# Two mixtures of experts after a short convolution: the first expert run in two parts, and the first layer of each mixture's first slot written ahead of the tables on TensorE

## The reference

```python
# convolution: x (4, 3584, 192), weight (8, 7), out reshaped to x (14336, 192)
out = np.einsum('hk,bskhg->bshg', w, x_unf)
# first mixture: w1 (8, 192, 1024), w2 (8, 1024, 192)
expert_idx = np.argmax(x @ w_gate, axis=1)
for e in range(E):
    mask = expert_idx == e
    out[mask] = gate_w[mask, None] * (np.maximum(x[mask] @ w1[e], 0.0) @ w2[e])
# second mixture, on the first one's output
noisy_logits = x @ w_gate + np.log1p(np.exp(x @ w_noise)) * noise
top2 = np.argpartition(-noisy_logits, 2, axis=1)[:, :2]
for e in range(E):
    for k in range(2):
        mask = top2[:, k] == e
        out[mask] += top2_w[mask, k, None] * (np.maximum(x[mask] @ w1[e], 0.0) @ w2[e])
```

## Time and profile before

| | |
|---|---|
| median of 3 runs | 1960.8 us (1959.62 to 1962.15) |
| the profiled execution | 1964.21 us, its span 1962.2 us |
| stage 1 | 0 to about 144 us |
| first mixture, second mixture | about 144 to 810 us, about 810 to 1962 us |
| PE busy over the span | 1876.2 us (96%) |
| DVE, POOL, ACT busy over the span | 65%, 49%, 47% |
| granted TensorE clock, mean | 0.982 of 2.4 GHz |

### The profile page before, as it was taken

How to read it: one execution, slowest core, us unless ns; L and a number is a source line. 1 busy time by engine, 2 the same in 40 slices (tenths; PEclk the granted TensorE clock), 3 DMA queues, 4 the chain that set the end, 5 groups by cost and what they waited for, 6 DMA issues and landing times.

```text
span 1962.2 us, 51451 instructions
## 1 busy us (share of the span) xinstructions
PE 1876.2 (96%) x14089; PEld 1821.5 (93%) x14090; DVE 1269.1 (65%) x4251; ACT 914.0 (47%) x2420; POOL 967.7 (49%) x1471
## 2 busy tenths in 40 slices
PE   8977599999999999799999999999999999999998
PEld 6657599999999999799999999999999999999998
DVE  5775488788887887655655655655655655655555
ACT  5543345555555455434444444444444444444444
POOL 4888554444444444444444444444444444444444
PEclk9979799999999999899999999999999999999999
DMA  7634243232332332322222222322322322322221
GB/s 274 230 113 128 74 127 120 89 115 79 117 118 84 116 100 92 103 74 62 81 78 62 85 74 62 104 63 63 102 62 64 96 64 66 97 62 86 78 63 48
DMA packets 113487, 185.23 MB, mean 94 GB/s; under 512 B 21675, under 2 KB 87971, under 8 KB 111287
## 3 DMA queue, kind: packets, MB, share of 16 engines
q1 hardware_dynamic: 73383, 104.53, 17.9%
q0 software_dynamic: 39936, 79.95, 12.6%
q10 hardware_dynamic: 144, 0.49, 0.1%
HBM read 111.34 MB, written 77.66 MB: 96 GB/s over the span
## 4 chain that ended last, share of the span: by engine, by line
PE 81%; issue 5%; DVE 5%; POOL 5%; ACT 1%; DMA 1%; DVEq 1%; ACTq 0%; POOLq 0%; SPq 0%
PE bank L1168 26%; PE bank L1169 12%; PE bank L1151 7%; PE bank L1153 7%; PE bank L1149 7%; PE bank L1152 7%; PE bank L1150 7%; POOL rows_of_mixture L1253 4%; PE bank L1138 2%; PE bank L1012 1%; DVE h_l L857 1%; PE bank L1139 1%; PE bank L1088 1%; POOL pause L1255 1%; DVE w1ml L666 1%
## 5 line engine op out<-in xcount | busy, mean ns | idle before, releaser
L1168 PE MATMUL bank<-w2hl,h_h 128*128 128x384 f32 (+1 forms) x2832 | 863.5, 370 | 14.4 <-DVE w2hl L672 6.7
L1169 PE MATMUL bank<-w2hl,h_l 128*128 128x192 f32 (+1 forms) x2832 | 721.1, 255 | 0.0
L857 DVE SCALAR_TENSOR_TENSOR h_l<-bank,h_h 128x512 fp32r<-128x512 f32 x708 | 477.5, 689 | 140.5 <-ACT h_h L565 101.2
L565 ACT ACTIVATE h_h<-bank 128x512 fp32r<-128x512 f32 x708 | 422.9, 598 | 301.2 <-PE bank L1153 261.6
L1168 PEld LDWEIGHTS bank<-w2hl,h_h 128*128 128x128 f32 x2832 | 534.0, 189 | 20.1 <-issue 12.6
L1169 PEld LDWEIGHTS bank<-w2hl,h_l 128*128 128x128 f32 x2832 | 543.1, 192 | 0.0
L1149 PE MATMUL bank<-x_h,w1mh 128*128 128x256 f32 x1416 | 401.7, 284 | 12.2 <-issue 9.5
L1280 POOL DMA_INDIRECT rows_of_mixture<-x_in,pos x248 | 245.7, 991 | 322.6 <-DVE h_l L857 110.0
L1151 PE MATMUL bank<-x_h,w1ml 128*128 128x256 f32 x1416 | 402.3, 284 | 0.5 <-issue 0.4
L1152 PE MATMUL bank<-x_h,w1lh 128*128 128x256 f32 x1416 | 400.1, 283 | 0.5 <-issue 0.5
L1153 PE MATMUL bank<-x_h,w1ll 128*128 128x256 f32 x1416 | 399.4, 282 | 0.2 <-issue 0.2
(11 more groups left out here) (199 smaller groups left out, 2017.0 us busy)
## 6 DMA issues: line engine op xcount, KB each, us to landing
rows<-rows_of_mixture SPq DMA_DIRECT2D x179, 208.0 KB
raw<-in_w_of_both SPq DMA_DIRECT2D x17, 1024.0 KB
raw<-in_w_of_both SPq DMA_DIRECT2D x17, 768.0 KB
out<-zeros SPq DMA_DIRECT2D x61, 192.0 KB
x_in<-in_x SPq DMA_DIRECT2D x15, 768.0 KB
raw<-in_moe_w_turned SPq DMA_DIRECT2D x8, 768.0 KB
rows_of_mixture<-pad_rows SPq DMA_DIRECT2D x21, 208.0 KB, 9.2
rows_of_mixture<-x_in,pos POOLq DMA_INDIRECT x248
```

Of the source, the lines that this page charges most:

```text
L565: nc.scalar.activation(h_h[:, 2 * p:2 * p + 2, :].rearrange("p c t -> p (c t)"), bank[1 + p][:], ACT.Relu).then_inc(hh_ready[m], 1)
L857: V.scalar_tensor_tensor(h_l[:, 2 * p:2 * p + 2, :].rearrange("p c t -> p (c t)"), bank[1 + p][:], 0.0, h_h[:, 2 * p:2 * p + 2, :].rearran ...
L1168: T.matmul(dst, h_h[:, c, tok], both, start=(c == 0), stop=False)
L1169: last = T.matmul(bank[5 + a][:, 0:width], h_l[:, c, tok], w2hl[:, c, 0:width], start=False, stop=(c == F // P - 1))
```

## The change

Expert 0 of the first mixture is worked in two parts: part 0 with its first slots, at most 4 (`FIRST_SLOTS`), at the head of the order, then experts 1 to 7, then part 8 with the rest of expert 0. With 6 slots of expert 0 the parts are 4, 8, 7, 9, 7, 7, 9, 8 and 2 slots, 61 as before. Expert 0's weights are loaded and split a second time for part 8. The `due` table covers the slots of experts 0 and 1 (16 entries), and SyncE uses it for both. The tables of the first mixture have 9 entries in place of 8, and a new table `part_row` tells SyncE at which row a part starts. The second mixture keeps its 8 experts. On TensorE, in both mixtures, `layer1` of slot 0 stands ahead of the wait for the tables, and the first part is written out ahead of the loop over the rest.

```diff
+EARLY_EXPERTS = 2
+FIRST_SLOTS = 4
+PARTS = [E + 1, E]
+PART0 = [0, E + 1]
...
-                with sp_.Fori(0, E) as e:
+                def row_of(part, highest):
+
+                    if m == 1:
+                        return part * CAP
+                    return sp_.value_load(part_row[0:1, bass.ds(part, 1)], min_val=0, max_val=highest)
+
+                with sp_.Fori(0, PARTS[m]) as e:
...
-                                with sp_.If(e * WORD + j < EARLY - 1):
-                                    slot_scattered((j + 1) % EARLY)
+                                with sp_.If(e // EARLY_EXPERTS * WORD + j < EARLY - 1):
+                                    slot_scattered((e * E + j + 1) % (EARLY_EXPERTS * E))
                                 with sp_.Else():
                                     all_scattered()
...
-                            load_rows(e * CAP + j * SLOT + SLOT)
+                            load_rows(row_of(e, (E - 1) * CAP) + j * SLOT + SLOT)
                         with sp_.Else():
                             if m == 0:
-                                all_scattered()
+                                with sp_.If(e < 1):
+                                    slot_scattered(E)
+                                with sp_.Else():
+                                    all_scattered()
...
-                            load_rows((e + 1) * CAP)
-                        g = E * m + e
+                            load_rows(row_of(e + 1, E * CAP))
+                        g = PART0[m] + e
+                        following = (e + 1) % E + e // E * (E - 1) if m == 0 else (E + e + 1) % (2 * E)
...
-                    V.tensor_copy(first_count[:, k:k + 1], bank[2][0:1, RANKS:RANKS + 1])
+                    V.tensor_copy(first_count[:, :, k], bank[2][0:1, RANKS:RANKS + EARLY_EXPERTS])
...
+                if m == 0:
+                    V.tensor_copy(part_row[:, 0:E], ecap[0:1, :])
+                    V.memset(part_row[:, E + 1:E + 2], E * CAP)
+                    V.tensor_scalar(slots[:, 1:E], t_shift[:, 1:E], 1.0, None, ALU.max)
+                    V.tensor_scalar(slots[:, E:E + 1], t_shift[:, 0:1], -float(FIRST_SLOTS), 1.0, ALU.add, ALU.max)
+                    link(V.tensor_scalar(t_first[:], t_shift[:, 0:1], -1.0, 1.0, ALU.add, ALU.max))
+                    link(V.tensor_scalar(slots[:, 0:1], t_first[:], float(FIRST_SLOTS), None, ALU.min))
+                    V.tensor_scalar(part_row[:, E:E + 1], slots[:, 0:1], float(SLOT), None, ALU.mult)
...
+                    second_half(s, e)
+
+                def second_half(s, e):
                     transpose_rows(s + 1)
                     for p in range(PAIRS):
                         layer2(s, e, p)
...
                 transpose_rows(0)
+                for p in range(PAIRS):
+                    layer1(0, 0, p)
                 pe.wait_ge(tables_ready[m], 1)
                 total = total_of(pe, m)
-                with pe.Fori(0, E) as e:
+                start, more = slots_of(pe, m, 0)
+                second_half(0, 0)
+                with pe.If(more > 0):
+                    with pe.Fori(1, more + 1) as j:
+                        body(j, 0)
+                with pe.Fori(1, PARTS[m]) as e:
```

More of the change, by code:

```diff
@@ L61 @@
 WORD = 64
-C_TOTAL = E
+C_TOTAL = E + 1
 def empty_tiles(c):
@@ L154, in attention_and_two_mixtures @@
         c_pos = sb("c_pos", [TILE, XROW, CHUNK], i32)
-        slots_in = sb("slots_in", [1, E])
-        first_count = sb("first_count", [1, DUE_COLUMNS])
+        slots_in = sb("slots_in", [1, EARLY_EXPERTS, E])
+        first_count = sb("first_count", [1, EARLY_EXPERTS, DUE_COLUMNS])
         slot_full = sb("slot_full", [1, E])
-        slot_in = sb("slot_in", [1, DUE_COLUMNS, E])
+        slot_in = sb("slot_in", [1, EARLY_EXPERTS, DUE_COLUMNS, E])
         late = sb("late", [1, 1], i32)
-        due = sb("due", [1, E], i32)
+        due = sb("due", [1, EARLY_EXPERTS * E], i32)
         count2 = sb("count2", [P, SUBS, E], bf16)
-        one = [sb(f"one_{m + 1}", [1, E + 2], i32) for m in range(2)]
+        one = [sb(f"one_{m + 1}", [1, E + 3], i32) for m in range(2)]
         t_cnt = sb("t_cnt", [1, E])
         t_int, t_shift = sb("t_int", [1, E], i32), sb("t_shift", [1, E], i32)
-        t_word = sb("t_word", [1, E])
-        t_cum = sb("t_cum", [1, 3, 2 * E + 1])
-        pad_at = [sb(f"pad_at_{m + 1}", [1, E + 1], i32) for m in range(2)]
+        t_word = sb("t_word", [1, E + 1])
+        t_cum = sb("t_cum", [1, 3, 2 * E + 3])
+        t_first = sb("t_first", [1, 1])
+        part_row = sb("part_row", [1, E + 2], i32)
+        pad_at = [sb(f"pad_at_{m + 1}", [1, E + 2], i32) for m in range(2)]
         raw1 = sb("raw1", [P, 2, F])
@@ L618, in _ @@
                 total = total_of(act, m)
-                with act.Fori(0, E) as e:
+                with act.Fori(0, PARTS[m]) as e:
                     start, more = slots_of(act, m, e)
@@ L789, in tables @@
                 link(V.tensor_copy(t_cnt[:], bank[6][0:1, 0:E]))
+                parts = PARTS[m]
                 V.tensor_tensor(pad_at[m][:, 0:E], t_cnt[:], ecap[0:1, :], ALU.add)
[L791 removed]
+                if m == 0:
+                    V.tensor_scalar(pad_at[m][:, E:E + 1], t_cnt[:, 0:1], float(SLOT), None, ALU.add)
+                V.memset(pad_at[m][:, parts:parts + 1], E * CAP).then_inc(pads_known[m], 1)
                 link(V.tensor_scalar(t_int[:], t_cnt[:], float(SLOT - 1), None, ALU.add))
@@ L793, in tables @@
                 link(V.tensor_scalar(t_shift[:], t_int[:], SLOT.bit_length() - 1, None, ALU.arith_shift_right))
[L794 to L799, removed]
@@ L800, in tables @@
-                link(V.scalar_tensor_tensor(t_word[:], before_e[:, 0:E], float(WORD), slots, ALU.mult, ALU.add))
-                V.tensor_scalar(one[m][:, 0:E], t_word[:], -1.0, None, ALU.add)
-                V.tensor_scalar(one[m][:, C_TOTAL + 1:C_TOTAL + 2], before_e[:, E:E + 1], -1.0, None, ALU.add)
-                V.tensor_copy(one[m][:, C_TOTAL:C_TOTAL + 1], before_e[:, E:E + 1]).then_inc(tables_ready[m], 1)
+                zero = E + 1
+                slots = t_cum[:, 0, zero + 1:zero + 1 + parts]
@@ new lines, in tables @@
+                if m == 0:
+                    V.tensor_copy(part_row[:, 0:E], ecap[0:1, :])
[5 more added lines that the diff above has]
+                    V.tensor_scalar(part_row[:, E:E + 1], slots[:, 0:1], float(SLOT), None, ALU.mult)
+                else:
+                    link(V.tensor_scalar(slots, t_shift[:], 1.0, None, ALU.max))
@@ new lines, in tables @@
+                end = zero + 1 + parts
+                turn = 0
+                for i, step in enumerate((1, 2, 4, 8)[:(parts - 1).bit_length()]):
+                    a, turn = t_cum[:, turn, :], (1, 2, 1, 2)[i]
+                    b = t_cum[:, turn, :]
+                    link(V.tensor_tensor(b[:, zero:end], a[:, zero:end], a[:, zero - step:end - step], ALU.add))
+                before_e = t_cum[:, turn, zero:end]
+                link(V.scalar_tensor_tensor(t_word[:, 0:parts], before_e[:, 0:parts], float(WORD), slots, ALU.mult, ALU.add))
@@ L804, in tables @@
+                V.tensor_scalar(one[m][:, 0:parts], t_word[:, 0:parts], -1.0, None, ALU.add)
+                V.tensor_scalar(one[m][:, C_TOTAL + 1:C_TOTAL + 2], before_e[:, parts:parts + 1], -1.0, None, ALU.add)
+                V.tensor_copy(one[m][:, C_TOTAL:C_TOTAL + 1], before_e[:, parts:parts + 1]).then_inc(tables_ready[m], 1)
                 return link
@@ L963, in _ @@
                 if m == 0:
-                    with dve.Fori(0, E) as e:
+                    with dve.Fori(0, PARTS[m]) as e:
                         start, more = slots_of(dve, m, e)
```

34 lines of the change are left out of this document (17 added, 17 removed).

## The result

The changed kernel takes 1931.52 us (median of 4, 1929.71 to 1935.05), where the kernel before takes 1961.47 in the same series (4 runs, 1959.62 to 1964.97): ratio 0.9847 with an interval of 0.9828 to 0.9867, a gain of 30 us. The prediction was 1945.0 with a range of 1938 to 1952.

A forecast was written before the change was run, and what follows sets the result against it. TensorE, 96% busy, stood idle from 192 to 216 us because slot 4 of expert 0 awaited GpSimd's whole scatter. 21.9 - 1.4 - 0.6 - 3.4 + 2.3 - 2.05 - 1.0 = 15.75 off 1960.8 gave 1945.0 us, range 1938 to 1952.

The forecast's parts named there:

- Step 5: One more weight switch, into part 8 at the first mixture's end: loss of 2.05 us.
- Step 7: SyncE's extra read in every slot of the first mixture: 0, or 0.5 us a slot if not covered.
- the rival of GpSimd's drain: Second mixture's scatter, started at 214, drains too slowly and becomes the bound: 1974 us, slower; chance 1 in 25.
- step 3: T(4) to T(5), transposes of slots 4 and 5, now under the scatter: 14.7 us instead of 11.25, loss 3.4.
- step 1: TensorE's hole before slot 4 goes: its transpose T(4) at 194.67 instead of 216.62, gain 21.9 us.
- The dear pace: Slots during GpSimd's stage 1 scatter came 14.99 and 14.36 us apart, against 10.0 later; taken as the stage's property.
- The rival of the whole hole: Dear pace comes from the first slots' starts and stops, not the scatter: 22 us gained, 1939 us; chance 1 in 8.
- Step 6: `layer1` of slot 0 ahead of the tables: loss 1.0 us, between +2 and -3, in the first mixture; 0 in the second.
- step 2: Switch moved to slots 3 and 4: loss 1.4 us for ScalarE's splits and 0.6 for VectorE's.
- step 4: Switch at slots 5 and 6 goes; T(6) to T(8) had taken 22.33 us: gain 2.3.

The follow-up runs named there:

- the version with early rows and four slots: Changed kernel with slot 1's rows loaded ahead of the tables and `layer1` ahead in the first mixture only, four slots in part 0: 1930.24 us, ratio 0.9845.

## Why the prediction was too small

**What was right.** TensorE's hole is what the change removes, and SyncE's long wait with it. Step 5, one switch more, was 2.05: T(59) to T(61) takes 22.06 us against 20.02 in the kernel before, 2.04. Part 8's weights just fit. Step 7, SyncE's extra read, was given 0, and no run tries it apart: the slots come 10.0 us apart, but see the last paragraph of this section. `store_rows` 0 is done at 222.26, ahead of T(8), so the rival of GpSimd's drain fell, but its slack was 3 us and not the 18 that I worked out, since body 7 came 15 us earlier than I thought. The drain, 222.26 to 269.51 for six slots, goes at 7.88 us a slot, where it was 7.93.

**What failed: step 3, and the T(4) of step 1, that "while GpSimd scatters stage 1, a slot is thus 4.7 us dearer".** The lead at T(8) should have been 17.8 us and was 33.8. Of the 16.0 us between them, 13.1 are T(4) (197.1 by the steps, 184.01 measured), 4.7 are T(4) to T(5) (15.3 against 10.62), and 1.6 go the other way, T(5) to T(6) (11.58 against 10.0, the second half of the switch). The dear pace belonged to one execution. The second profile of the kernel before has the same scatter, the same order and 10.0 us a slot, and its time differs from the first's by only 2.5 us: the hole behind it absorbed the delay. The 13.1 at T(4) come apart like this: the prediction carried three dear steps, 14.99, 14.36 and, in the relu of body 3 at 193.54, a third of 14.15 from T(3) to T(4), 13.5 us above 10.0 each; the 1.4 for ScalarE's splits doesn't show at T(4) (T(3) to T(4) is 9.97); and 1.6 go the other way, since `layer1` ahead cost 2.6 and not 1.0. I had read the earlier trace rows in a stretch with slack, where a slot's pace says nothing of the end, and made it a cost in a kernel that has no slack there. The rival of the whole hole, to which I gave 1 in 8, came nearest with its 1939 us, but it was right only in that the scatter doesn't make the pace. Its own cause, the starts and stops of the first slots, isn't shown: the other profiles have the same starts and no dear slots. It left T(2) and T(3) where the first profile had them, and it added 1.5 us for a `layer1` ahead that costs. A sign was there to be read: the earlier trace rows puts the wait down to remote behind matmuls recorded as done, and nothing in the trace tied that late word to the scatter but the time at which it stood.

**Step 6** was given -1.0 between +2 and -3. It measured -2.6 at T(2); for the second mixture, where I had 0, no cost is shown. The medians differ by 2.5 and 3.7 (1930.41 and 1931.52 against 1927.87, in other series). Its mechanism was right: TensorE idles 5.1 us with `layer1` done, and starts again cold. I had sized the restart by a single slot behind the hole, 1.25 us, and credited the relus. That slot came from the first profile as well: T(4) to T(5) is 11.25 there, and 12.39 and 12.45 in the two later profiles of the same kernel, 2.4 above 10.0, which is what the restart costs here. The granted clock from 219 to 222 us was 0.95 in the first, and 0.61 and 0.50 in the later ones. The Trainium skill warns in TensorE: Matmul & The Clock Gate, "Why this matters for your kernels", that an idle gap between bursts of matmuls drops the clock to its lower level; the gap of 5.1 us here and the run without it agree, by 2.7 us at T(2).

**Steps 2 and 4** were right in size: the switch stands at T(4) to T(6) and costs 10.62 + 11.58 - 20.0 = 2.2 us there, where step 2 had 1.4 + 0.6, and T(6) to T(8) takes 20.15 us instead of 22.33, 2.2 where step 4 had 2.3. Only the place of the 1.4 was wrong, behind T(4) and not ahead of it.

**What the medians add.** The lead of 33.8 at T(8) falls to 31.8 at T(59), since 51 slots take 10.07 and 9.97 in turn, 10.28 with the switches, against 10.24 before. The seven profiles of kernels with four or five slots in part 0 take 523.2 to 524.4 us for these 51 slots, the four of kernels without parts 521.5 to 522.3. SyncE's read of `part_row` stands in each of these slots and is a candidate, so step 7 may have cost some 2 us; no run leaves it out, and the cause is open. T(65) is 26.4 us ahead, as T(64) to T(65) takes 13.48 us there against 10.77; then the lead grows to 32.0 at the last transpose, since the first profile of before has seven more slots of 10.7 to 11.3 us in the second mixture and the changed kernel has none above 10.5 behind T(65). Against the second profile of before the lead is 32.2 at T(4), 34.6 at T(8), 26.8 at T(65) and 29.9 at the end. The spans differ by 32.4 in the first pair, by 31.1 in the second (1928.5 against 1959.6), the medians by 30.

## What to carry to other kernels

A stretch that ends in a long wait doesn't tell its own pace: what is slow in it costs nothing now, and before it is taken into a new plan, it needs a second execution or the same work seen elsewhere. The price of a restart, taken from the same execution, was too small by half as well. To start work earlier pays only if what comes next on the same engine is there too; a piece moved ahead of a wait leaves its gap behind it, and here the gap cost a restart at the lower clock, 2.6 us, until the next slot's load was moved along. When a loop is cut in two to fill a hole, look at the short end too: a part of one slot had no time to bring in the next weights, which cost 8.5 us.

## What the runs showed of the hardware

- One profiled execution of three of an unchanged kernel ran two slots in 14.99 and 14.36 us, with ScalarE and VectorE waiting for something remote while the matmuls that they needed were recorded as done. The two later ones ran them in 9.98 and 10.02, and in 10.01 and 11.35. No other profile of this case has such a wait, and its cause is open.
- GpSimd's indirect scatter did not slow under a busy VectorE: 9.63 of 12 us with VectorE at 0.95 us (second profile of before, 180 to 192) and at 10.96 (changed kernel, same window).
- An idle stretch of TensorE of 5.1 us was followed by a granted clock of 0.50 (152 to 155 us), and with 24 matmuls of 128x512 in it the clock there was 1.00. An idle stretch of 4.1 us, in the version with early rows and four slots, was followed by 0.50 too (171 to 174 us). Each such restart cost 2.2 to 2.7 us of a slot.
